# Attention and two MLPs on one core: the order of one load on the sync queue, and the step at which the first MLP groups begin

## The reference

```python
# 1: block-causal attention, batch 4, 8 heads, 576 tokens, head size 64, blocks of 64 tokens
scores = scale * q @ k.T ; masked where block_i < block_j
attn = softmax(scores) ; x = attn @ v                  # -> x: 2304 x 512
# 2: a dense MLP, 512 -> 2048 -> 512
h = x @ w_in ; g = maximum(0.01 * h, h) ; x = g @ w_out
# 3: a gated mixture of 8 experts (512 -> 1024 -> 512), one expert for each token, plus x
```

## Time and profile before

| | |
|---|---|
| median of three runs | 754.63 us |
| the profiled execution, its own time | 755.92 us |
| its span in the profile | 754.2 us |
| TensorE matmul busy | 738.7 us, 98% of the span |
| VectorE / ScalarE / GpSimd busy | 359.4 / 296.5 / 145.2 us |
| granted TensorE clock, mean | 0.998 |
| share of the chain that ended last on TensorE | 92% |

### The profile page before, as it was taken

One profiled execution on the slowest core, in us unless ns is written; L12 is line 12 of the kernel. 1 busy time (PEld: TensorE's weight loads), 2 busy tenths in 40 slices (PEclk: granted clock), 3 DMA queues, 4 the chain that ended last, 5 costly groups with the idle time before them and its releaser, 6 DMA issues.

```text
span 754.2 us, 12647 instructions
## 1 busy us (share of the span) xinstructions
PE 738.7 (98%) x4358; PEld 595.4 (79%) x4359; DVE 359.4 (48%) x761; ACT 296.5 (39%) x674; POOL 145.2 (19%) x190
## 2 busy tenths in 40 slices
PE   7999999999999999999999999999999999999997
PEld 4555778778887887898888788878787879999984
DVE  5777454464446452012345455565655352352641
ACT  5566665455455543234422212232221131342550
POOL 3136554232213321100020000000000032212221
PEclk9999999999999999999999999999999999999999
DMA  4345777554555522475666566666653116767773
GB/s 128 96 123 160 208 205 223 144 152 129 159 149 143 153 86 71 112 195 171 194 188 192 156 192 165 191 174 169 184 157 96 57 43 220 253 214 243 224 229 101
DMA packets 97537, 121.60 MB, mean 161 GB/s; under 512 B 13842, under 2 KB 60706, under 8 KB 97480
## 3 DMA queue, kind: packets, MB, share of 16 engines
q1 hardware_dynamic: 94664, 116.50, 52.9%
q0 software_dynamic: 1920, 3.77, 1.6%
q10 hardware_dynamic: 896, 0.59, 0.3%
HBM read 89.09 MB, written 31.31 MB: 160 GB/s over the span
## 4 chain that ended last, share of the span: by engine, by line
PE 92%; DVE 2%; issue 2%; DMA 2%; ACT 1%; POOL 1%; SPq 0%; DVEq 0%; POOLq 0%; ACTq 0%
PE ps_h L1728 9%; PE ps_x L1810 9%; PE ps_x L1812 9%; PE ps_x L1811 9%; PE ps_hid L1982 9%; PE ps_h L1730 8%; PE ps_h L1729 8%; PE ps_o L1711 6%; PE ps_t L1685 4%; PE ps_y L1993 2%; PE ps_y L1995 2%; PE ps_y L1994 2%; PE ps_s L1673 2%; PE ps_s L1672 2%; PE ps_s L1636 2%
## 5 line engine op out<-in xcount | busy, mean ns | idle before, releaser
L1728 PE MATMUL ps_h<-xh,win_h 128*128 128x512 f32 (+1 forms) x320 | 124.1, 388 | 3.7 <-ACT act L1084 2.8
L1730 PE MATMUL ps_h<-xh,win_l 128*128 128x512 f32 (+1 forms) x320 | 118.3, 370 | 0.0
L1729 PE MATMUL ps_h<-xl,win_h 128*128 128x512 f32 (+1 forms) x320 | 118.1, 369 | 0.0
L1810 PE MATMUL ps_x<-wout_h,g_hi 128*128 128x512 f32 x288 | 114.0, 396 | 0.0
L1812 PE MATMUL ps_x<-wout_h,g_lo 128*128 128x512 f32 x288 | 112.3, 390 | 0.0
L1811 PE MATMUL ps_x<-wout_l,g_hi 128*128 128x512 f32 x288 | 112.1, 389 | 0.0
L1070 ACT ACTIVATE prob<-ps_s,neg_max 128x128 f32<-128x128 f32 (+3 forms) x144 | 79.0, 550 | 59.3 <-DVE neg_max L1291 42.3
L1291 DVE TENSOR_REDUCE neg_max<-ps_s 128x1 f32<-128x128 f32 (+3 forms) x144 | 71.2, 509 | 58.0 <-PE ps_s L1673 36.5
L1084 ACT ACTIVATE act<-ps_h 128x512 f32<-128x512 f32 (+1 forms) x80 | 44.3, 555 | 117.1 <-PE ps_h L1730 113.5
L1331 DVE TENSOR_TENSOR g_lo<-g_raw,g_hi 128x512 fp32r<-128x512 f32 x72 | 49.5, 687 | 58.2 <-ACT g_hi L1094 58.0
L1728 PEld LDWEIGHTS ps_h<-xh,win_h 128*128 128x128 f32 x320 | 60.3, 189 | 15.9 <-issue 5.6
(11 more groups left out here) (205 smaller groups left out, 1096.9 us busy)
## 6 DMA issues: line engine op xcount, KB each, us to landing
g_raw<-hidden SPq DMA_DIRECT2D x72, 256.0 KB, 3.8
hidden<-act SPq DMA_DIRECT2D x64, 256.0 KB, 2.4
w_sb<-in_w SPq DMA_DIRECT2D x32, 512.0 KB, 4.9
w_two<-in_w SPq DMA_DIRECT2D x32, 512.0 KB, 5.0
k_raw<-in_k_t SPq DMA_DIRECT2D x40, 144.0 KB, 3.1
x2rows<-x SPq DMA_DIRECT2D x18, 256.0 KB, 2.4
out<-x SPq DMA_DIRECT2D x18, 256.0 KB, 2.6
w_stage<-in_w_in SPq DMA_DIRECT2D x16, 256.0 KB, 3.2
```

What stands on the lines that cost most here:

```text
L1728: e.matmul(dst, win_h[:, f, kc, :], xh[m][:, kc, :], start=kc == 0, stop=False)
L1729: e.matmul(dst, win_h[:, f, kc, :], xl[m][:, kc, :], start=False, stop=False)
L1730: last = e.matmul(dst, win_l[:, f, kc, :], xh[m][:, kc, :], start=False, stop=kc == KC - 1)
L1810: e.matmul(dst, hi, wout_h[:, f, :], start=f == 0, stop=False)
```

## The change

Two edits. First, part p of group g (g below 16) moves from step `50 + 34 * (2g + p) // 32` to step `51 + 33 * (2g + p) // 32`. Group 0 now stands in steps 51 and 52, group 1 in 53 and 54, up to group 7 in 65 and 66. Step 50 has no hidden part any more, and step 66 has one. Groups 8 to 15 keep their steps. For the groups 0 to 7, part 0 moves from an even to an odd step, and `copy_hidden` of these groups moves with part 1 from ScalarE's even steps (52 to 66) to its odd steps (53 to 67).

Second, on SP the loads of the odd head's queries are issued behind the copy of the even head's rounded keys, not at place 2 behind the odd head's keys. This concerns heads 13, 15, ... 31, so it occurs ten times, in all pairs from 5 to 14. No transfer is added or taken away.

```diff
             if g < FC:
-                s = 50 + 34 * (2 * g + part) // (2 * FC)
+                s = 51 + 33 * (2 * g + part) // (2 * FC)
             elif g < 2 * FC:
...
                     if i == 2 and ROW_PAIRS <= p + 1 < N_PAIRS:
                         load_head_k(e, 2 * p + 3)
-                        load_head_q(e, 2 * p + 3)
                     if hi == 3 and ROW_PAIRS <= hp + 1 < N_PAIRS:
                         copy_k(2 * hp + 2)
+                        load_head_q(e, 2 * hp + 3)
```

## The result

The changed kernel is slower. In the comparison it took 756.4 us (median of 20 runs, 754.88 to 757.71) against 755.14 us for the kernel before (20 runs, 753.94 to 756.53): ratio 1.0018, 95% interval 1.0012 to 1.0025, so +1.4 us (0.9 to 1.9); the two medians differ by 1.3. The profiled execution took 756.18 us with a span of 754.4, against 755.92 and 754.2. The forecast was 0.3 us faster.

What follows compares the result with a forecast made beforehand. TensorE, busy 98% of the span, was taken as the bound, so only its waits count. Terms -0.88, -1.15, +1.44, +0.3 and 0 gave -0.3 us: 754.3 us from the 754.63 median, range 752.9 to 756.9.

Steps and rivals of the forecast that it cites:

- Part 1: Step 50 loses its hidden part, so step 52 starts 2.35 us earlier, 1.47 of it only put off: -0.88 us.
- Part 2: Steps 58 and 62 no longer wait for ScalarE's copy out of the PSUM bank: 0.46 and 0.69, together -1.15 us.
- Part 3: Steps 53, 61 and 63 now wait for that bank, each needing 0.95 us between parts: +1.44 us.
- Part 4: Around steps 54 and 55, group 1's copy queues behind `high_x`, whose spread inverse comes 2.2 us earlier: +0.3, between 0 and 0.66.
- Part 5: Later pairs, query loads behind the rounded keys: hidden, taken as 0; upper bound 0.9 us for each of two heads.
- Rival A: At step 55 the inverse's store stays slow and group 2 starts at 83.95: +2.3 us, 756.9; chance 0.15.
- Rival C: Late query loads hold the rounding engines at two heads: net +1.5 us at most, likelier +0.6, 755.2; chance 0.12.

Runs made afterwards that it cites:

- e4: Kernel before with only the first MLP group moved, whole into step 51, and query loads moved only up to pair 8: 754.39 against 754.77 us.
- e9: Kernel before with only the first halves of groups 4 and 6 one step later (58 to 59, 62 to 63): 753.57 against 754.84 us.
- e5: The changed kernel run again, nothing altered: 756.69 us against 755.48 for the kernel before, ratio 1.0025.
- e6: Changed kernel with ScalarE's rounding of x behind the copy of the hidden group from step 88 on: 755.87 us against 755.48 for the kernel before.
- e3: Kernel before with both edits, but query loads behind the rounded keys only up to pair 8: 755.47 against 754.77 us, ratio 1.0005.
- e7: Changed kernel with group 0's copy ahead of two load-waiting roundings in step 53: 757.36 us against 755.48 for the kernel before.
- e2: Kernel before with the second edit alone, MLP parts at their old steps: 755.35 against 754.77 us, ratio 1.0014.
- e12: The kernel before, unchanged, profiled once more: 755.96 us.
- e13: The kernel before, unchanged, a second further look: 756.82 us.
- e1: Kernel before with the first edit alone, query loads still ahead of the rounded keys: 755.9 against 754.77 us, ratio 1.0013.
- e14: The kernel before, unchanged, a third further look: 754.03 us.

## Why the prediction was wrong, point by point

**Part 1 (-0.88).** The sum was right for the profile it was made from (e4: -0.94, the lead at step 52 2.28). Of the seven waits in the earlier trace rows only two (0.21 and 0.56) lie in the steps that the change moves; the largest wait there was the 0.81 for GpSimd, and the whole part hung on it. It failed as a gain: 0.81 of it is the wait in the earlier trace rows, and two of the four profiles of the kernel before have no such wait. Without it, step 50 without its hidden part is worth e4's -0.94 against -0.86, about 0.1 us. I took a wait of one execution for a property of the kernel, although that execution was 1.3 us above its own median and I had said so. With four looks at the kernel before (front 0, -0.04, -0.86, -0.86: mean -0.44) what step 50 is worth on average shrinks to -0.94 + 0.44 = -0.50.

**Part 2 (-1.15).** Right. e9 measured 0.46 + 0.72 by the stages and -1.2 us by the clock. (The third of the later steps with this distance is 79, which lies in pair 8 and not in pair 7; it has 0.94.)

**Part 3 (+1.44).** The mechanism was right, and step 61 has its 0.94 (steps 60, 62 and 66 together came out 0.3 us better than the terms say). Step 53 was mis-sized: 1.60, 1.50, 1.86 and 2.13 in the four profiles with both edits (changed, e5, e6, e3), not 0.95. I had read the 0.95 in steps in which ScalarE was idle, and allowed 0.23 above it. In step 53 the copy stands behind two roundings that wait for loads. TensorE is 2.3 us earlier, and on the clock of the kernel before the last query load went out 0.7 later (69.95 against 69.25) and landed 1.7 later (73.22 against 71.53). The mis-sized 0.65 costs nothing of its own, though, as part 4 takes in whatever is lost before step 55 (e7).

**Part 4 (+0.3).** This is the step that failed in the front: that the store would be through 1.78 us after its issue, as in the earlier trace rows. The spread was forecast near 72.3 and came at 72.88 + 0.57 = 73.45 on the clock of the kernel before, 1.0 earlier than before and not 2.2 (73.6 to 73.9 in e5, e6 and e3). It went out 0.2 us behind the landing of the last query load, and that took 3.3 and 3.4 us in the changed kernel and e5, where the one in the earlier trace rows took 2.3. The store's own long issue (1.50) did not matter: with 0.50 in e5 the spread was no earlier. The rest of the chain gave back 1.0: the last part of the spread landed after 2.9 and not 3.6 us, and the normalisation took 1.42 and not 1.62. So group 2 started at 81.95, and at 82.3 to 82.6 in e5, e6 and e3: 0.9 to 1.5 behind the 81.09 at which TensorE was to be ready, where I took 0.3 and at most 0.66. Rival A (pinned to the normaliser's chain) has the right mechanism and too high a price: the front is held at step 55, at 82.0 to 82.6 and not at 83.95. e7 shows that it is a pin: 0.65 won in step 53 was lost in step 55. No run put the store ahead of the query loads, so that it is their landing which holds the spread is read from the traces and not shown by an edit.

**Part 5 (0).** This is the step that failed in kind, as I put at nothing a wait that I had not looked at. "No TensorE instruction waited for any of these" was true of the kernel before, and I drew the bound from the query loads alone. What the edit made late in the later pairs was the spread of the inverse behind them: 2.15 us late, slack 2.05, and 0.41 to 0.49 on TensorE at pair 14 in both profiles of the changed kernel, 0.43 at pair 10 as well in two variants (e2, e7; there the normalisation took 1.81 and 1.93 and not 1.43). I had listed the spread as queued behind and never asked for its slack. Rival C (late queries) is refuted by e6.

**The sum as measured.** The fronts of the four profiles with both edits are -0.11, +0.60, +0.34 and +0.41, mean +0.31; those of the kernel before have a mean of -0.44. The difference, 0.75, and 0.45 at pair 14 make 1.2 us, against +1.2 and +1.3 by the medians of the two comparisons. That they meet so closely is in part luck, since the mean of the kernel before rests on four looks, two with the wait and two without. The stages from 191 to 200 and from 323 to 400 us and the offset at 60 us differ as much between looks at one kernel as between kernels, and I count them as noise. The measured time lies within the stated range of 752.9 to 756.9, but that range reached so far for rival A with a store as slow as before, and it was not (2.86 for 3.95); the way was forecast wrong.

The Trainium skill's rule on completion order, weighed under part 4 (page "DMA: Bandwidth & Descriptors", section "Queues, rings and completion order"), would have given 2.3 for this part, with a landing of 4.0. The traces agree with the rule: in all 16 profiles the spread of pair 4 went out 0.20 to 0.23 us after the last landing among the transfers issued ahead of the store, while the time from the store's issue to the spread ran from 1.97 to 3.95., which I had held against it, agrees as well (178.51 and 178.62). I had given the rule's way a small chance for want of one look, at the landing of the query loads in the earlier trace rows. It is not strict for whole transfers: of the 114 spreads behind 60 us before which SP stood idle for over 0.15 us, in all 16 profiles, five went out 0.03 to 1.35 before that landing, the other 109 within 0.24 after it.

## What to carry to other kernels

Before a term is built on a wait, see it in a second profile: a wait of 0.8 us that one late load decides is in some executions and not in others, and an execution that lies above its median may well hold such a one. When a wait is for a transfer, look at the landing of what was issued ahead of it, and not only at its own time. When something is moved back in a queue, take the slack of everything that it is now in front of, in every repetition of the loop, and follow each to what stands behind it in the consumer's own order. Where one bank is handed back and forth, put both halves of a group into the step behind the short one: it costs no wait, and here each such move gave 0.45 to 0.72 us.

## What the runs showed of the hardware

- VectorE's cast of the keys takes 0.46 us when it starts before GpSimd's subtraction and 1.45 when it starts 0.13 behind it (e12, e13); the rest of x on GpSimd takes 1.55 or 2.13. That agrees with the Trainium skill, page "SBUF — State Buffer", section "Who interferes with whom": the two engines share a pair of ports, the first to issue has it for its whole instruction, and the other stands still. The page names copies and casts among what can take it; the length of the stall, 1.45 - 0.46 = 0.99 us here, is near what was left of GpSimd's instruction (64.59 + 1.27 - 64.72 = 1.14). In all 16 profiles the cast took 0.46 in the 13 in which it started first, and 1.45 to 1.53 in the three in which it started 0.05 to 0.13 behind.
- TensorE lost 0.9 to 1.2 us near 191 us in e3, e7, e12 and e13, and not in the other twelve profiles. In e12, SP's copy of the rounded keys, TensorE, and the landing of that copy (line 697 alone in its window):

```profile
187.37 0.52 SPq L697 DMA_DIRECT2D k<-k_st  x1
...
191.61 0.78 PE L1662 MATMUL ps_s<-k_st,q_hi 128*128 128x288 f32 x4 [0.95 <-issue]
...
DMA to landing us min/median/max: 4.2/4.2/4.2
```

  The profile names "issue", as in e1, but these scores need the copied rounded keys, and TensorE went on 0.09 to 0.10 us after these had landed in all four profiles (e12: 191.52 and 191.61). There the copy took 3.7 to 4.2 us to land, in the other twelve 2.6, which is 0.3 to 0.6 us before TensorE wants it. Just behind the copy, SP took 2.74 us to issue two loads that take 1.25 elsewhere (187.93 to 190.67; e3: 2.55). The wait is not tied to an edit, since the kernel before has it in two of four looks. Why the copy lands late stays open. Together with the wait of the first hidden part it makes 1.8 of the 2.8 us between e13 (756.82) and e14 (754.03), two executions of one kernel, so a gain of 0.3 is lost in any single run.
- A wait for a transfer can stand under "issue" in the list of waits: 1.44 us in e1 and 0.69 to 0.95 in these four. The landing of the transfer, 0.09 us before the instruction, tells it.
